# Feed-forward layers for two blocks of tokens at a time with w_in as the stationary operand; the low part of x^T on GpSimd; new orders on all engines

## What is computed

```python
def _attn_ref(q, k, v):                       # batch 2, 8 heads, 576 positions, head size 64
    scores = scale * np.matmul(q, k.transpose(0, 1, 3, 2))
    kth = np.partition(scores, -top_k, axis=-1)[..., -top_k:-top_k + 1]     # top_k = 32
    mask = scores >= kth
    scores = np.where(mask, scores, -1000000000.0)
    attn = np.exp(scores - np.max(scores, axis=-1, keepdims=True))
    attn = attn / (np.sum(attn, axis=-1, keepdims=True) + 1e-09)
    return np.matmul(attn, v)

def _moe_ref(x, w_in, w_out, alpha):          # x 1152 x 512, w_in 512 x 2048, w_out 2048 x 512
    h = x @ w_in
    g = np.maximum(h, 0.0) + alpha * np.minimum(h, 0.0)
    return g @ w_out

def _moe2_ref(x, w_gate, w_noise, noise, w1, w2):   # 8 experts, hidden size 1024
    noisy_logits = x @ w_gate + np.log1p(np.exp(x @ w_noise)) * noise
    # the two best experts of each token, softmax of the two as weights, then for expert e:
    #   out[mask] += top2_w[mask, k, None] * (np.maximum(x[mask] @ w1[e], 0.0) @ w2[e])
```

## Time and profile before

| | |
|---|---|
| median of 3 runs | 758.88 us (757.73 to 762.43) |
| the profiled execution | 760.67 us, of which the span from the first to the last instruction 758.9 us |
| PE busy, matmuls / loads | 664.5 us (88%) / 564.7 us (74%) |
| DVE, ACT, POOL busy | 521.5 us (69%), 465.2 us (61%), 392.8 us (52%) |
| the chain that ended last, by engine | PE 70%, POOL 11%, DVE 5%, ACT 4%, issue 4%, DMA 4% |
| DMA | 140.95 MB, mean 186 GB/s |

### The profile page before, as it was taken

How to read it: one execution, slowest core, us unless ns; L and a number is a source line. 1 busy time by engine, 2 the same in 40 slices (tenths; PEclk the granted TensorE clock), 3 DMA queues, 4 the chain that set the end, 5 groups by cost and what they waited for, 6 DMA issues and landing times.

```text
span 758.9 us, 13760 instructions
## 1 busy us (share of the span) xinstructions
PE 664.5 (88%) x4660; PEld 564.7 (74%) x4660; DVE 521.5 (69%) x1103; ACT 465.2 (61%) x878; POOL 392.8 (52%) x435
## 2 busy tenths in 40 slices
PE   2467767999989999999999998369999999999993
PEld 2355656887867888888887777258989989989992
DVE  5799997888779989898989043454555554555520
ACT  5588866777887777777877545614554544535511
POOL 3488899678788677776787634400202202202112
PEclk9987998999999999999999999759999999999998
DMA  9759446643507536244644749380638448366222
GB/s 307 309 185 414 132 167 210 236 169 141 217 17 268 183 127 239 99 192 154 249 140 174 278 182 385 148 291 1 188 118 277 130 160 275 93 213 208 88 32 35
DMA packets 39607, 140.95 MB, mean 186 GB/s; under 512 B 10800, under 2 KB 11824, under 8 KB 35504
## 3 DMA queue, kind: packets, MB, share of 16 engines
q1 hardware_dynamic: 35168, 130.25, 47.5%
q0 software_dynamic: 4384, 9.98, 5.8%
HBM read 113.70 MB, written 45.73 MB: 210 GB/s over the span
## 4 chain that ended last, share of the span: by engine, by line
PE 70%; POOL 11%; DVE 5%; issue 4%; ACT 4%; DMA 4%; POOLq 0%; ACTq 0%; SPq 0%; DVEq 0%
PE bank L1125 12%; PE bank L974 11%; PE ps_scores L1111 9%; PE bank L935 7%; PE bank L1111 6%; PE bank L912 6%; PE bank L1130 4%; PE bank L940 3%; PE ps_scores L865 3%; POOL expo L1567 3%; PE bank L896 3%; DMA q_raw<-q_rows_dram 2%; PE bank L952 2%; DVE top L414 2%; PE bank L1093 1%
## 5 line engine op out<-in xcount | busy, mean ns | idle before, releaser
L1709 POOL DMA_INDIRECT out_dram<-ye,xe x24 | 42.8, 1783 | 219.1 <-ACT ye L1475 214.2
L414 DVE MAX8 top<-rest 128x8 f32<-128x576 f32 x216 | 152.2, 745 | 0.0
L1567 POOL TENSOR_TENSOR expo<-scores,expo 128x576 f32<-128x576 f32 x72 | 103.6, 1440 | 68.1 <-ACT scores L1195 68.0
L426 DVE MATCH_REPLACE8 rest<-top,rest 128x576 f32<-128x576 f32 x144 | 105.7, 741 | 0.0
L974 PE MATMUL bank<-w_out_high,g_parts 128*128 128x512 f32 x288 | 100.2, 410 | 0.0
L1125 PE MATMUL bank<-w_hi,he_t 128*128 128x512 f32 x256 | 91.9, 400 | 0.0
L604 DVE TENSOR_TENSOR w_lo<-raw,w_hi 128x1024 fp32r<-128x1024 f32 x64 | 77.8, 1225 | 19.5 <-ACT w_hi L1419 18.4
L912 PEld LDWEIGHTS bank<-v,prob_t 128*64 128x64 f32 (+1 forms) x1440 | 57.4, 145 | 30.2 <-ACT prob_t L1222 15.6
L912 PE MATMUL bank<-v,prob_t 128*64 128x65 f32 (+1 forms) x1440 | 73.1, 241 | 5.8 <-ACT prob_t L1222 5.8
L414 DVE MAX8 top<-scores 128x8 f32<-128x576 f32 x72 | 52.6, 746 | 33.7 <-ACT scores L1161 33.3
L935 PE MATMUL bank<-w_in_parts,x_t 128*128 128x512 f32 x272 | 71.2, 405 | 2.2 <-DMA w_in_parts<-w_parts_dram 2.2
(11 more groups left out here) (192 smaller groups left out, 1606.3 us busy)
## 6 DMA issues: line engine op xcount, KB each, us to landing
w_in_parts<-w_parts_dram SPq DMA_DIRECT2D x16, 2048.0 KB, 7.9
raw<-w_dram SPq DMA_DIRECT2D x64, 512.0 KB, 10.8
x_sorted_dram<-x_sorted_dram SPq DMA_DIRECT2D x7, 2570.0 KB, 10.9
w_parts_dram<-w_in_parts SPq DMA_DIRECT2D x4, 2048.0 KB, 10.1
q_raw<-q_rows_dram SPq DMA_DIRECT2D x18, 256.0 KB, 5.0
xe<-x_sorted_dram SPq DMA_DIRECT2D x8, 514.0 KB, 4.6
w_in_raw<-w_in_dram SPq DMA_DIRECT2D x4, 1024.0 KB, 11.0
w_out_raw<-w_out_dram SPq DMA_DIRECT2D x4, 1024.0 KB, 15.8
```

Source lines behind the costliest of these rows:

```text
L414: nc.vector.max(dst, src).then_inc(chain if r < ROUNDS - 1 else dve_top, 1)
L426: nc.vector.match_replace(rest[:, k, :], top[:, (n + k) % 4, 8 * r:8 * r + 8], src, LOWEST).then_inc(chain, 1)
L1567: nc.gpsimd.tensor_tensor(expo[:, n % 4, :], scores[:, n % SBUFS, :], expo[:, n % 4, :], ALU.mult).then_inc(pool_prob, 1)
```

## The change

- **Two blocks at a time.** Blocks (0,1), (2,3), (4,5), (6,7) form four duos; block 8 goes alone. Duo d runs through the net while attention is in blocks 2d+2 and 2d+3, in 8 units of 256 hidden units. So nothing of the net is in block 1 any longer, and of the last duo only four of eight first halves and two second halves stand inside attention (block 8); TAIL_UNIT and what follows stand behind it.
- **w_in stationary.** `first_layer` now loads a 128x128 piece of w_in and moves x^T of both blocks, 256 columns: 24 matmuls for a unit, 192 for a duo. Its result already has hidden units as its rows, so `copy_h1` and `h_transpose` are gone for the duos; block 8 keeps the old form (`last_first`, `last_turn`).
- **Second layer** for a unit: 12 matmuls of 512 columns, 6 for each block, into two banks (ps_y, ps_y2).
- **Low x^T on POOL.** POOL has no way to the bank here, so ACT makes two copies of it (the high part and a plain one, `xf`), and POOL subtracts (`low_x`); PE's first unit waits for `pool_xt`. For a duo both `low_x` stand in step 1 of an even block, the second one behind the threshold.
- **Orders.** On POOL the threshold now stands behind `low_g` and the weight pieces of its step. All eight low pieces of w_out are POOL's (two were DVE's). The splitting of w_in is in steps 0 to 13 and that of w_out in steps 4 to 24; keys of the second batch start at steps 9 and 13. On ACT the ReLUs of a unit stand ahead of `copy_prob_t`. w_in is loaded again once for a duo: 10 reloads of 2 MB in place of 16. The third chunk of w_in is no longer ahead of block 1's queries on SP's list. The score buffers are 6 in place of 8; EARLY is 6, and blocks 6 and 7 are routed together.

The diff, cut (the first `low_x` is DVE's, the second POOL's; `copy_x_t` is ACT's; the last piece is PE's list behind the last block of attention):

```diff
-SBUFS = 8
+SBUFS = 6
-EARLY = BLOCKS - 2
+EARLY = BLOCKS - 3
+UNITS = 8
+DUOS = BLOCKS // 2
+TAIL_UNIT = UNITS * (DUOS - 1) + 4
+FIRST_AT = {1 + 2 * u: u for u in range(UNITS)}
+SECOND_AT = {4 + 2 * u: u for u in range(UNITS - 2)}
+REST_SECOND_AT = {0: 6, 2: 7}
...
-            def low_x(j):
-                dve.wait_ge(act_xt, j + 1)
-                nc.vector.tensor_tensor(x_t[:, 1, :, :]..., ps_t[:, :], x_t[:, 0, :, :]..., ALU.subtract)
...
-            def first_layer(j, c, dst=ps_h[:, :], alone=False):
-                for k in range(MK):
-                    for b in range(2):
-                        pe.matmul(dst, x_t[:, 0, k, :], w_in_parts[:, c % 2, b, k * 512:(k + 1) * 512], ...)
-                if c == 0:
-                    pe.wait_ge(dve_xt, j + 1)
-                for k in range(MK):
-                    mm = pe.matmul(dst, x_t[:, 1, k, :], w_in_parts[:, c % 2, 0, k * 512:(k + 1) * 512], ...)
+            def first_layer(d, u, dst=ps_h[:, :], lag=0):
+                if u == 0:
+                    pe.wait_ge(act_xt, 2 * d + 2)
+                wait(pe, act_relu, UNITS * d + u - lag)
+                for i in range(2):
+                    for k in range(MK):
+                        for b in range(2):
+                            pe.matmul(out_of[:, i, :], w_of[b][:, k, at[i]], x_parts(0, k), ...)
+                    if u == 0:
+                        pe.wait_ge(pool_xt, 2 * d + 2)
+                    for k in range(MK):
+                        mm = pe.matmul(out_of[:, i, :], w_of[0][:, k, at[i]], x_parts(1, k), ...)
...
-            def h_transpose(j, c, dst=ps_t, src=h_sb[:, :], banks=1):
...
+            def second_layer(d, u):
+                for t, y in enumerate((ps_y, ps_y2)):
+                    for i in range(2):
+                        m = unit_tile(d, u) + i
+                        for a, w in ((0, w_out_high), (0, w_out_low), (1, w_out_high)):
+                            at = (2 * i + t) * P
+                            mm = pe.matmul(y[:, :], g_parts[:, u % 2, a, at:at + P], w[:, m * MODEL:(m + 1) * MODEL], ...)
...
+            def copy_x_t(j, src=ps_h):
+                nc.scalar.copy(x_t_of(j, 0), src[:, :].rearrange("p (k n) -> p k n", k=MK))
+                nc.scalar.copy(xf[j % 2], src[:, :]).then_inc(act_xt, 1)
...
+            def low_x(j):
+                pool.wait_ge(act_xt, j + 1)
+                nc.gpsimd.tensor_tensor(x_t_of(j, 1), xf[j % 2]..., x_t_of(j, 0).bitcast(F32), ALU.subtract).then_inc(pool_xt, 1)
...
+            second_layer(d, 2)
+            first_layer(d, 4)
+            x_transpose(j, ps_pt)
+            second_layer(d, 3)
+            first_layer(d, 5, unit_h[1], lag=1)
+            second_layer(d, 4)
+            last_first(0)
+            rank(0, ps_pt4)
+            first_layer(d, 6, lag=1)
+            second_layer(d, 5)
+            first_layer(d, 7, unit_h[1], lag=1)
+            last_turn(0)
+            second_layer(d, 6)
+            last_first(1)
+            second_layer(d, 7)
...
```

More of the change, by code:

```diff
@@ L473, in _ @@
             first_low_keys(1)
-            one_block(0, True)
-            one_block(1, second=True)
-            one_block(2)
-            one_block(3)
-            one_block(MIXED, mixed=True)
-            one_block(MIXED + 1, after_mixed=True)
-            with dve.Fori(MIXED + 2, BLOCKS) as blk:
+            for blk in range(BLOCKS):
                 one_block(blk)
             row_sums(BLOCKS - 1, 1)
-            low_x(BLOCKS - 1)
             steps = [0]
@@ L542, in place_early, with place_two @@
                 step(v3.tensor_tensor(base[:, :], origin[:, :], upto[:, :, BLOCKS - 1], ALU.add))
+            def place_two(b, turn, bank):
+                dve.wait_ge(pe_rank, turn + 1)
+                n = 2 * EXPERTS
+                ranks, counts = (bank[:, k * n:(k + 1) * n].rearrange("p (e b) -> p e b", e=EXPERTS) for k in range(2))
+                for i in range(2):
+                    step(v3.tensor_tensor(x_place_two[:, :, i], ranks[:, :, i], base[:, :], ALU.add))
+                    step(v3.tensor_tensor(base[:, :], base[:, :], counts[:, :, i], ALU.add))
+                for k in range(2):
+                    step(v3.tensor_tensor(hot_two[:, k, :, :], hot[:, k, :, b:b + 2], x_place_two, ALU.mult), hold=(k == 1))
+                step(v3.tensor_reduce(slot_f[:, :, b:b + 2], hot_two.rearrange("p k e b -> p k b e"), AX.X, ALU.add))
+                step(v3.tensor_copy(slot_i[:, :, b:b + 2], slot_f[:, :, b:b + 2]), f"slots{turn}")
             def place_block(b, turn, bank):
@@ new lines, in last_first @@
+            def last_first(c):
+                if c >= 2:
+                    pe.wait_ge(w_in_back[c % 2], 16 * DUOS + 16)
+                if c == 0:
+                    pe.wait_ge(act_xt, BLOCKS)
+                    pe.wait_ge(pool_xt, BLOCKS)
+                if c == 1:
+                    pe.wait_ge(act_o, 2 * BLOCKS)
+                if c >= 2:
+                    pe.wait_ge(act_relu, UNITS * DUOS - 3 + c)
+                for k in range(MK):
+                    for a, b in ((0, 0), (0, 1), (1, 0)):
+                        mm = pe.matmul(last_h[c], x_t_last[:, a, k, :], w_in_parts[:, c % 2, b, k * 512:(k + 1) * 512],
+                                       start=(k == 0 and a == 0 and b == 0), stop=(k == MK - 1 and a == 1))
+                mm.then_inc(pe_first_last, 1)
@@ L1049, in _ @@
[L1049 to L1058 removed]
+            for blk in range(2, BLOCKS - 1):
+                one_block(blk)
+            one_block(BLOCKS - 1, last=True)
+            d, j = DUOS - 1, BLOCKS - 1
@@ L1649, in _ @@
+            one_block(0)
             pool.wait_ge(small_in, 48)
```

912 lines of the change are left out of this document (480 added, 432 removed).

## The result

The median of the changed kernel is 783.62 us (783.52 to 786.15, 4 runs); the kernel before, run beside it, took 760.65 (757.73 to 765.44). The ratio is 1.0304, 95% interval 1.0242 to 1.0365: slower by 3%. The forecast was 748 with a range of 736 to 762.

A forecast was written before the change was run, and what follows sets the result against it. Attention was taken as bound by PE's list, DVE close behind. Block 2 starting at 106 plus 300.5 us for blocks 2 to 8 ends attention at 406.5 (-28.5); +18 behind it leaves about -11: 758.9 - 11 = 748 us, range 736 to 762.

The forecast's parts named there:

- Prices: Times of PE's pieces: a unit of 24 256-column matmuls takes 2.86 us; 32 units cost +3.5 us (bounds -7, +16).
- second sum: Check by PE's work alone: -17 + 3.5 - 2.2 + 2.1 x 3 is -9.6 us, said to agree.
- Rival D: In `first_layer`, loads of w_in pieces set the pace: 769 us at 147 ns a matmul, +74 at 215; chance 0.12.
- Step 1: Turns of h on PE: 32 of 36 go, at 0.53 us each, -17 us where PE bounds.
- Step 2: Block 1: queries land 3.3 us earlier and attention runs alone, so block 2 starts at 106, not 118: -12 us.
- Step 3: Block 2: PE has only 34 us of work, POOL 40.9 and some idle, so the block takes 42.5 us.
- Steps 4 and 5: Blocks 3 to 8, odd then even, from PE's work and holds: 43, 46.8, 39.7, 45.2, 39.7, 43.6 us.
- the prediction's own signs: Wrong if: 256-column matmul over 135 ns, block 2 after 112, odd block 43 us, PE's ACT/DVE waits behind attention over 8.
- hold of 2.1 us for `low_x`: Step 1 of even blocks: the first unit's second half waits for POOL's second `low_x`, +2.1 us a block.
- rival C: DVE and PE don't average out; later thresholds may keep odd blocks at 43, or start gains 3: 756 to 758; chance 0.28.
- Step 7: Behind attention: PE has 56.9 us of work plus 4 of waits, 61 us, +18 on the 43 before.
- Step 8: Nothing for fewer reloads, six score buffers, DVE's freed low x^T and four scatters, which if late cost up to 5 us.

The follow-up runs named there:

- e2: e1 plus alpha's product and sum one step after their ReLU, `g_high` behind `copy_scores` on ACT and `low_g` a step later: 748.69 us.
- e1: The changed kernel with a pair's threshold directly behind the product of its odd step on POOL, ahead of `low_g` and w_out pieces: 777.39 us.
- e3: The changed kernel without POOL's alpha product and sum for the first eight blocks, `g_high` waiting for the ReLU alone: 752.25 us.
- e4: The changed kernel with ten unused 512-column matmuls on PE in each of steps 9 to 18: 784.76 us.

## Why the prediction was wrong

- **Prices: right.** The forecast was 24 matmuls of 256 columns in 2.86 us. Chain of the changed kernel, last step of block 6:

```profile
357.89 0.92 PE bank L999 x8
358.81 0.45 PE bank L1004 x4
359.26 0.91 PE bank L999 x8
360.17 0.45 PE bank L1004 x4
```

  2.73 us, 114 ns each (119 said), so the 768 matmuls cost what the 384 of twice the width did, and not 3.5 us more. (The lower bound of that term is -11 us by the prediction's own prices, not -7, and its second sum gives -9.4, not -9.6; neither moves the forecast.) Rival D is out: the loads of these matmuls last 203 ns by the profile and lie beside the matmuls before them. The estimate that the prediction made from the Trainium skill (TensorE: Matmul & The Clock Gate, "LDWEIGHTS (loading the stationary operand)" and "Part 3: Packing small matmuls", The mechanism), 213 ns each, doesn't agree with this trace. What the prediction quoted was also incomplete: "The mechanism" says too that a load into the background weight buffer is pulled ahead of running matmuls, and with that the trace agrees (114 ns from one matmul to the next, with a load before each).
- **Step 1, the turns: right**; e2's blocks 5 and 7 are full of PE work and take 39 and 40 us (39.7 forecast).
- **Step 2, the start: right in direction, 3 us short.** Block 2 starts at 109 (106 forecast, 118 before). Block 1's queries land 14.8 us after their issue (16.9 before, 13.6 forecast), and block 1 begins at 68.0 for 69.2. It then lasts 40.8 us; with the threshold back in front it lasts 38.6, and block 2 starts at 106.8 (e1) and 106.3 (e2). The clock sank to 0.62 in block 1, as considered, and didn't hold up DVE (40.5 of 41 us busy).
- **Step 3, block 2: the step that failed.** It added POOL's work to 40.9 us (40.73 in the window, right) and took a block of 42.5 for that. The block took 56.4. A sum over a block can't see that POOL took 10.5 us from one product to the next in one step, nor that 3.2 of them were a wait for a ReLU that PE had just made possible. With the order of e2 the same work fits: block 2 took 42.9.
- **Steps 4 and 5, blocks 3 to 8: the same failure**, +12.2, +4.6, +2.8, +2.9, +1.7 and -1.2. Blocks 2 to 4 suffer most; pieces of w_out and keys stand in their steps. By the prediction's own signs it is wrong here: an odd block takes 55.2 us (block 3, 43 forecast), and blocks 5 and 7 take 42.5 and 41.4. The hold of 2.1 us for `low_x` in each even block isn't borne out as such: block 6 of e2 takes 44.6, forecast 45.2, but PE's wait for x_t is 0.5 us in it, 1.7 over four blocks (2.4 in the changed kernel). Of the 35 us that e2 wins back in blocks 2 to 8, 23 are PE's idle time behind the alphas; the rest, the threshold (6 by e1) and the slower clock among it, isn't split.
- **What was left out.** The prediction weighed the threshold's place (rival C, up to 10 us; e1 measured 6) and `low_x`, both seen in the diff, and never asked of `prelu` in which step the ReLU stands that it waits for: the sum has no term for that wait, which measured 51.3 us on POOL and 26.2 us of PE's idle time. "What is queued behind it, and who waits" was answered for `low_x` alone. No rival held this case: the one on the slower side was another mechanism.
- **Step 7, behind attention: 57 us**, 61 forecast, 56 of them busy on PE: the four us of waits that I kept have gone to one.
- **Step 8, costed at nothing: right as far as it shows.** Behind attention PE waits for one thing, 1.0 us for DVE's low part, and for no reload; routing and experts are the same to half a us.

The sum of the other steps is near what e2 shows: 748.7 us against the 748 forecast. That doesn't make the forecast right; it was made for a kernel whose POOL never waits for a ReLU. Nor is it as close as it looks: in e2 blocks 2 to 8 take 302 us (300.5 forecast) and the stretch behind attention 57 (61), and these misses offset each other.

## What to carry to other kernels

In a pipeline written out as lists, look at each piece on the engine that serves the critical product, and ask in which step the work stands that it waits for. If it is the same step, the next product is behind it and a loop through three engines is closed; put it a step later than what it waits for, and check that for each hop (ReLU, alpha, high part, low part), since one hop moved alone can close another. A block's sum of busy time doesn't tell whether an engine keeps up (40.7 us of POOL in a block that took 56.4), and neither does the sum of its waits (77.0 us in the fast e3). The longest stretch between two products doesn't either: the fast e2 has one of 8.5 us in block 2 and another of 9.7 later. What told it in these runs is who arrives first: compare when the product ends with when the bound engine reaches its use, step by step.

## What the runs showed of the chip that I had not expected

- Matmuls of 256 columns with their own 128x128 load go at 114 ns, 5 ns less than the line from 320 and 512 columns gave (119). That is 0.45 ns a column, the same as for 512 (229 ns).
- The granted clock follows the stalls: 0.82 in block 2 of the changed kernel, 0.93 in e2's. Window behind the stall of 5.8 us of step 18:

```profile
131.50:134.00 2.50, 2.43 (x11) 2.40 (x12) 2.50 (x7) 0.94 (x3) 2.04 (x6) 0.50 0.00 0
```

  The granted clock there is 0.50, the lower of its two levels (1.2 GHz), and the four transposes took 1.12 us; after a wait of 0.2 us in block 6, at a clock of 1.00, they took 0.66. So a long stall costs twice: its own length and slower work behind it. Filling PE's idle time with other work (e4) raised the clock to 0.91 and gained nothing, since the loop stayed.
